# One wait per matmul: semaphore waits of TensorE dropped, moved to an earlier matmul, or moved to VectorE

## The reference: what is computed

```python
def _attn_ref(q, k, v):                       # q, k, v: 4 x 8 x 576 x 64
    scores = scale * np.matmul(q, k.transpose(0, 1, 3, 2))
    scores = np.where(mask, scores, -1000000000.0)   # block_i >= block_j, blocks of 64
    scores = scores - np.max(scores, axis=-1, keepdims=True)
    attn = np.exp(scores)
    attn = attn / (np.sum(attn, axis=-1, keepdims=True) + 1e-09)
    return np.matmul(attn, v)

def _moe_ref(x, w_in, w_out):                 # x: 2304 x 512, w_in: 512 x 2048
    h = x @ w_in
    g = np.where(h >= 1, h, np.where(h <= -1, 0.0, (h + 1) ** 2 / 4))
    return g @ w_out

def _moe2_ref(x, w_in, w_out):
    h = x @ w_in
    return (h * np.cos(h)) @ w_out
```

## Time and profile before

| | |
|---|---|
| median of 3 runs | 1044.91 us (1044.8 to 1045.8) |
| the profiled execution, its own time | 1051.79 us |
| its span, first to last instruction | 1049.6 us |
| PE busy | 1001.9 us, 95% of the span |
| DVE, ACT, POOL busy | 657.0, 590.8, 426.5 us (63%, 56%, 41%) |
| mean granted TensorE clock | 0.981 |

### The profile page before, as it was taken

How to read it: one execution, slowest core, us unless ns; L and a number is a source line. 1 busy time by engine, 2 the same in 40 slices (tenths; PEclk the granted TensorE clock), 3 DMA queues, 4 the chain that set the end, 5 groups by cost and what they waited for, 6 DMA issues and landing times.

```text
span 1049.6 us, 19879 instructions
## 1 busy us (share of the span) xinstructions
PE 1001.9 (95%) x7360; PEld 943.1 (90%) x7360; DVE 657.0 (63%) x1422; ACT 590.8 (56%) x1232; POOL 426.5 (41%) x446
## 2 busy tenths in 40 slices
PE   4688999999999999999999999999999999999997
PEld 3578999999999999999999998999999999999995
DVE  5567777766766767666732378656565555656553
ACT  5567776766666666666633356544444444445442
POOL 3559765555555554655522221222222222222211
PEclk9579999999999999999999999999999999999999
DMA  4335321221211212121200144010110101001000
GB/s 133 104 118 157 98 90 65 72 70 49 92 49 53 89 49 72 70 72 65 69 31 22 41 161 162 1 40 0 40 40 0 40 0 40 21 19 40 0 21 21
DMA packets 30886, 62.28 MB, mean 59 GB/s; under 512 B 3680, under 2 KB 11872, under 8 KB 30816
## 3 DMA queue, kind: packets, MB, share of 16 engines
q1 hardware_dynamic: 29664, 57.16, 17.1%
q10 hardware_dynamic: 1152, 4.19, 1.1%
HBM read 51.90 MB, written 9.44 MB: 58 GB/s over the span
## 4 chain that ended last, share of the span: by engine, by line
PE 79%; DVE 9%; ACT 5%; issue 3%; POOL 1%; DMA 1%; ACTq 0%; POOLq 0%; DVEq 0%
PE hidden L1090 33%; PE acc L1107 18%; PE acc L1115 12%; PE heads_out L1036 4%; PE scores L1001 4%; PE turned L1019 3%; PE scores L1002 3%; DVE neg_max L800 1%; PE heads_out L1019 1%; DVE x_lo L879 1%; PE hidden L1073 1%; DVE wout_lo L865 1%; DVE work L885 1%; ACT probs L616 1%; DVE pt_lo L817 1%
## 5 line engine op out<-in xcount | busy, mean ns | idle before, releaser
L543 POOL TENSOR_TENSOR g_lo<-work,g_hi 128x512 fp32r<-128x512 f32 x144 | 187.9, 1305 | 450.7 <-ACT g_hi L713 450.7
L1090 PE MATMUL hidden<-x_hi,win_hi 128*128 128x256 f32 x1136 | 323.5, 285 | 2.8 <-DVE work L912 1.2
L1090 PE MATMUL hidden<-x_hi,win_lo 128*128 128x256 f32 x1136 | 317.9, 280 | 0.0
L1090 PE MATMUL hidden<-x_lo,win_hi 128*128 128x256 f32 x1136 | 317.9, 280 | 0.0
L1090 PEld LDWEIGHTS hidden<-x_hi,win_hi 128*128 128x128 f32 x1136 | 214.3, 189 | 7.6 <-issue 2.0
L1090 PEld LDWEIGHTS hidden<-x_lo,win_hi 128*128 128x128 f32 x1136 | 214.2, 189 | 3.3
L1090 PEld LDWEIGHTS hidden<-x_hi,win_lo 128*128 128x128 f32 x1136 | 216.4, 190 | 0.0
L1115 PE MATMUL acc<-g_hi,wout_hi 128*128 128x256 f32 x576 | 167.4, 291 | 0.3 <-ACT y_stage L696 0.3
L1115 PE MATMUL acc<-g_lo,wout_hi 128*128 128x256 f32 x576 | 160.6, 279 | 0.0
L1115 PE MATMUL acc<-g_hi,wout_lo 128*128 128x256 f32 x576 | 160.5, 279 | 0.0
L513 POOL TENSOR_SCALAR probs<-probs,row_inv 64x576 f32<-64x576 f32 (+2 forms) x160 | 107.4, 675 | 121.6 <-DVE row_inv L812 120.8
(11 more groups left out here) (91 smaller groups left out, 1830.1 us busy)
## 6 DMA issues: line engine op xcount, KB each, us to landing
qk_raw<-qk_late SPq DMA_DIRECT2D x32, 448.0 KB, 3.2
qk_raw<-qk_early SPq DMA_DIRECT2D x32, 256.0 KB, 2.6
v_raw<-v_late SPq DMA_DIRECT2D x32, 160.0 KB, 3.3
x_raw<-x_scratch SPq DMA_DIRECT2D x9, 512.0 KB, 3.5
out<-y_stage SPq DMA_DIRECT2D x36, 128.0 KB, 2.4
x_raw<-w_in SPq DMA_DIRECT2D x8, 512.0 KB, 3.6
y_stage<-w_out SPq DMA_DIRECT2D x8, 512.0 KB, 3.5
x_scratch<-y_stage ACTq DMA_DIRECT2D x8, 512.0 KB, 2.7
```

Source lines behind the costliest of these rows:

```text
L543: nc.gpsimd.tensor_tensor(g_lo[:, m % G_RING, :], work[:, m % 2, :], g_hi[:, m % G_RING, :], ALU.subtract).then_inc(g_lo_made, 1)
L1090: last = nc.tensor.matmul(into, w[:, p, c, half * P:(half + 1) * P], x[:, c, :], start=(i == 0), stop=(i == len(products) - 1))
```

## The change

Three kinds of edits, all of them about which instruction waits for what. No computing instruction is added, removed or put elsewhere.

1. Waits that another one implies are left out on PE: `score` waits for `q_lo_made` at its first tile only, and no longer for `k_lo_made`; instead DVE waits for `k_lo_made` ahead of `split_q`, so that `q_lo_made` tells of both. The waits for the exponential remain at the third tile, and at the first where the order of the slots does not imply them (`banks_seen`).
2. Waits of `turn_b` and `turn_c`, of `make_hidden` (for `hidden_read`) and of `use_hidden` (for `g_lo_made`, `wout_lo_made`) move to one or two matmuls ahead of where they stood; `heads_read` and `v_lo_made` move from `weigh` to the transposes in part.
3. In the second layer the waits for each half of the weights (`half_lo_made`) are reduced to the last half that is made.

```diff
@@ split_q, DVE @@
             def split_q(n):
+
+                dve.wait_ge(k_lo_made, n + 1)
                 dve.wait_ge(q_hi_made, n + 1)
@@ score, PE @@
-                pe.wait_ge(q_lo_made, n + 1)
-                pe.wait_ge(k_lo_made, n + 1)
-
-                if late(n):
-                    pe.wait_ge(exp_made, first_tile(n) + (2 if i == 4 else 0))
-                elif n > ALONE:
-                    pe.wait_ge(exp_made, first_tile(n - 1) + e + 1)
-                elif n > 1:
-                    pe.wait_ge(exp_made, first_tile(n - 1 if n < ALONE else n))
+
+
+                if e == 0:
+                    pe.wait_ge(q_lo_made, n + 1)
+                    if not banks_seen(n):
+                        pe.wait_ge(exp_made, first_tile(n))
+                elif e == 2:
+                    pe.wait_ge(exp_made, first_tile(n) + 2)
@@ turn, PE @@
-                if e == 1:
-                    pe.wait_ge(heads_read, n)
-                elif e == 2:
-                    pe.wait_ge(pt_lo_made, first_turn(n) + 1)
-                elif user_before(n) >= 0:
-                    pe.wait_ge(pt_lo_made, first_turn(user_before(n) + 1))
...
+                    if not late(n) and c == 1 and user_before(n) >= 0:
+                        pe.wait_ge(heads_read, user_before(n) + 1)
+                    if kind(n) == 1 and c == 2:
+                        pe.wait_ge(v_lo_made, n + 1)
...
+            def turn_ahead(n, k):
+
+                for m, j in near(n, k):
+                    if late(m) and j == slot_of("turn_b", m):
+                        pe.wait_ge(heads_read, m)
+                    if late(m) and j == slot_of("turn_c", m):
+                        pe.wait_ge(pt_lo_made, first_turn(m) + 1)
+
             def weigh(n):
+
+
                 pe.wait_ge(pt_lo_made, first_turn(n) + (3 if late(n) else 1))
-                pe.wait_ge(v_lo_made, n + 1)
-                if user_before(n) >= 0:
-                    pe.wait_ge(heads_read, user_before(n) + 1)
+                if kind(n) == 0:
+                    pe.wait_ge(v_lo_made, n + 1)
@@ make_hidden, PE @@
-                if half == 0:
-                    pe.wait_ge(hidden_read, PAIRS * t + m + 1)
...
+                    if i == len(products) // 2 - 1:
+                        ahead_of_half(beside, 2 * u)
...
+                    if i == len(products) - 2 and ahead is not None:
+                        ahead()
+                    if i == len(products) - 1:
+                        ahead_of_half(beside, 2 * u + 1)
@@ tile, PE @@
-                    if second and (u % 4 == 0):
-                        for h in range(2):
-                            if s == 0:
-                                pe.wait_ge(half_lo_made[0][h], PAIRS - 1)
-                                pe.wait_ge(half_lo_made[1][h], PAIRS - 2)
-                            if s == PAIRS - LAG - 1:
-                                pe.wait_ge(half_lo_made[0][h], PAIRS)
-                            if s == PAIRS - 2:
-                                pe.wait_ge(half_lo_made[1][h], PAIRS)
+
+
+                    if second and u == 4 * (PAIRS - LAG - 1):
+                        pe.wait_ge(half_lo_made[1][1], PAIRS - 1)
+                    if second and u == 4 * (PAIRS - LAG) + 1:
+                        pe.wait_ge(half_lo_made[1][1], PAIRS)
```

More of the change, by code:

```diff
@@ L113, in user_before, with banks_seen @@
     return n - 2 if n < ALONE else n - 1
+def banks_seen(n):
+    before = n - 2 if n < ALONE else n - 1
+    last = "inv_c" if late(before) else "inv_b"
+    return n < 2 or slot_of(last, before) - sum(slots_of(m) for m in range(before, n)) <= slot_of("q_lo", n)
 def near(n, k):
@@ L1008, in turn @@
                 pe.wait_ge(probs_made, first_tile(n) + e + len(tiles))
-                if e == 1:
-                    pe.wait_ge(heads_read, n)
-                elif e == 2:
-                    pe.wait_ge(pt_lo_made, first_turn(n) + 1)
-                elif user_before(n) >= 0:
-                    pe.wait_ge(pt_lo_made, first_turn(user_before(n) + 1))
                 at = 0
-                for i, j in ([(0, 0), (1, 0), (1, 1)] if not late(n) else [(tiles[0], j) for j in range(tiles[0] + 1)]):
+                chunks = [(0, 0), (1, 0), (1, 1)] if not late(n) else [(tiles[0], j) for j in range(tiles[0] + 1)]
+                for c, (i, j) in enumerate(chunks):
                     q = rows_of(i)
+                    if not late(n) and c == 1 and user_before(n) >= 0:
+                        pe.wait_ge(heads_read, user_before(n) + 1)
+                    if kind(n) == 1 and c == 2:
+                        pe.wait_ge(v_lo_made, n + 1)
                     last = nc.tensor.transpose(turned_of(n, e)[:, at:at + q], probs_chunk(n, i, j), ident[0:q, 0:q])
@@ L1063, in beside_half, with ahead_of_half @@
                         attention(n, k)
+            def ahead_of_half(beside, half):
+                if beside:
+                    for n, k in beside[half]:
+                        turn_ahead(n, k)
             def begin_hidden(c):
@@ L1077, in begin_hidden, with hidden_ahead, use_ahead, make_hidden @@
                         last.then_inc(hidden_made, 1)
-            def make_hidden(t, m, half, beside=None, u=0):
+            def hidden_ahead(t, m):
+                pe.wait_ge(hidden_read, PAIRS * t + m + 1)
+            def use_ahead(t, p, first):
+                if p == 0:
+                    pe.wait_ge(g_lo_made, PAIRS * t + p + 1 + 2)
+                elif first:
+                    pe.wait_ge(wout_lo_made, p + 1)
+            def make_hidden(t, m, half, beside=None, u=0, ahead=None):
                 p = m % PAIRS
-                if half == 0:
-                    pe.wait_ge(hidden_read, PAIRS * t + m + 1)
                 into = hidden[:, m % H_BANKS, half * TOK:(half + 1) * TOK]
@@ L1093, in make_hidden, with use_hidden @@
                     last.then_inc(hidden_made, 1)
-            def use_hidden(t, p, half, second, beside=None, u=0):
-                if half == 0:
+            def use_hidden(t, p, half, second, beside=None, u=0, ahead=None):
+                if half == 0 and p == 0:
+                    pe.wait_ge(acc_read, t + 1)
+                elif half == 0:
                     pe.wait_ge(g_lo_made, PAIRS * t + p + 1 + 2)
-                    if p == 0:
-                        pe.wait_ge(acc_read, t + 1)
                 slot = p % G_RING
@@ L1105, in use_hidden @@
                         for i, (w, g) in enumerate(parts):
+                            if a == 1 and i == 1 and ahead is not None:
+                                ahead()
                             at = half * TOK + a * P
@@ L1113, in use_hidden @@
                         for i, (w, g) in enumerate(parts):
+                            if d == KC // 2 - 1 and i == 2:
+                                ahead_of_half(beside, 2 * u)
+                            if d == KC - 1 and i == 1 and ahead is not None:
+                                ahead()
+                            if d == KC - 1 and i == 2:
+                                ahead_of_half(beside, 2 * u + 1)
                             into = acc[:, d // 2, (d % 2) * TOK:(d % 2 + 1) * TOK]
@@ L1123, in tile, with ahead_of @@
                 heads = beside is not None
+                first = heads and t == 0
+                def ahead_of(u):
+                    s = u // 4
+                    if u == UNITS:
+                        return (lambda: hidden_ahead(t + 1, LAG)) if next_tile else None
+                    if u == made_at(s, heads) - 1 and (s + LAG < PAIRS or next_tile):
+                        return lambda: hidden_ahead(t, s + LAG)
+                    if u == (made_at(s, heads) + 1 if made_at(s, heads) == 4 * s + 1 else 4 * s) and (first or s == 0):
+                        return lambda: use_ahead(t, s, first)
+                    return None
                 for u in range(UNITS):
@@ L1138, in tile @@
                             if to_second and m >= PAIRS and half == 0:
-                                for h in range(2):
-                                    pe.wait_ge(half_lo_made[0][h], m - PAIRS + 1)
-                            if heads and t == 0 and m < PAIRS and half == 0:
+                                pe.wait_ge(half_lo_made[0][1], m - PAIRS + 1)
+                            if first and m < PAIRS and half == 0:
                                 pe.wait_ge(win_lo_made, m + 1)
-                            make_hidden(t, m, half, beside, u)
+                            make_hidden(t, m, half, beside, u, ahead_of(u + 1))
                     else:
-                        if heads and t == 0 and half == 0:
-                            pe.wait_ge(wout_lo_made, s + 1)
-                        use_hidden(t, s, half, second, beside, u)
+                        if first and s == 0 and half == 0:
+                            pe.wait_ge(wout_lo_made, 1)
+                        use_hidden(t, s, half, second, beside, u, ahead_of(u + 1))
```

(2 more changed lines are left out.)

## The result

The changed kernel takes 1146.06 us in the median of 4 runs (1144.07 to 1151.93), the kernel before 1044.86 us. The ratio is 1.0975, with a 95% interval of 1.0949 to 1.1001: 101 us slower, where 60 were forecast and 1130 us was the upper end of the range. The direction, the place and the size of the stall were right; the number of the clock's falls and the cost of a wait moved in the early items were not.

A forecast was written before the change was run, and what follows sets the result against it. PE was taken to bound the kernel, busy 1001.9 of 1049.6 us. Stalls 54.7 + early items 2 + clock 8 - saved waits 4 = 60.7 us, on the median 1044.9, gave 1105.6, said as 1105; range 1070 to 1130.

The forecast's parts named there:

- Part 1, "DVE stands still for 2.5 us": In each late item DVE stands still 2.5 us ahead of `split_q`, waiting for `k_lo`; near 75 us in the sum.
- a fixed price: DVE's 2.5 us stop, two POOL instructions of 1.04 + 1.41 us, is paid 32 times, once in every late item.
- Part 1, "18 x 2.1 + 13 x 1.3 = 54.7 us": PE's stalls at 31 pairs of late items: 18 lose 2.1 us in the mean, 13 lose 1.3.
- Part 1, the early items, 2 us for `k_lo`: In items 0, 15, 21 and 32 the score starts about 0.5 us later each: 2 us.
- Part 2, "I take 5, 8 us": PE's clock falls behind 5 of the stalls in late items, 1.6 us each: 8 us added.
- rival A: Same stalls in late items, but the clock falls at all 31, 50 us in place of 8: 1147 us, chance 8%.
- Part 3, moved waits at 0: PE's waits moved by one or two matmuls, and `heads_read` moved from `weigh` to the transposes, cost 0.
- Part 3, 4 us saved: In late items seven separate PE waits of 51 ns go or join weight loads: 4 us saved, at most 11.4.
- The sum's own base: The profiled execution, 1051.8 us, would become 1112.5; the median of the runs stands 6.9 us lower, at 1044.9.

The follow-up runs named there:

- only_k: The kernel before with one edit: DVE's `split_q` waits for `k_lo_made` and PE's `score` no longer does; 1126.80 us, ratio 1.0783.
- q_late: The changed kernel with `split_q` of late items put behind `pt_lo` in DVE's order, the wait for `k_lo_made` staying on DVE; 1071.57 us.
- the undoing runs: The changed kernel with the `k_lo_made` wait back on PE, 1055.67 us; also early `v_lo_made` back at `weigh`, 1047.35; also `heads_read`, 1045.72.
- the two fill runs: The changed kernel with ten or five added matmuls ahead of each `turn_c`'s wait for `pt_lo`; 1123.64 us with ten, 1130.05 us with five.
- before_again: The kernel before, unchanged, profiled a second time; an execution of 1045.34 us.

## Why the prediction was right in kind and wrong in size

- **Part 1, "DVE stands still for 2.5 us"**: right. 32 times, 76.2 us in the sum (near 75 forecast), 2.4 us in the mean, released by `k_lo`. That it is "a fixed price" was wrong: `normalise` got 0.28 us shorter (last section).
- **Part 1, "18 x 2.1 + 13 x 1.3 = 54.7 us"**: right. PE's wait for `pt_lo` grew from 2.0 to 55.9 us, its time not busy by 51.7; in `only_k` it waits 54.8 us, 31 times. `q_late` shows that the path is the one named, through `pt_lo`. That the sum comes out so close is partly luck, since the shorter `normalise` and the later start of the score behind `pt_lo` cancel (0.3 us each in item 53).
- **Part 1, the early items, 2 us for `k_lo`**: small, as said. `only_k` has 126 us there against 125.
- **Part 2, "I take 5, 8 us"**: this step failed, the term of the sum for the clock. It took 43 us: 21 falls in the late items, four of them of double length, so 25 times the 1.7 us that a fall costs. The price was about right (1.6 forecast, though its own working, 14 x 3.41 / 32, gives 1.5). The number was wrong: it was reached by counting only stalls of 2.0 us and more and then taking a third of them. Once the items no longer run alone the trace of before has one fall, and from one fall no shortest length can be read. In the changed kernel all eight stops of PE of 2.0 us and more bring a fall, and so do 14 of the 19 from 1.3 to 2.0 us. The match of 1146 with rival A's 1147 is partly chance: A had 50 us of clock and none of the 10 us of the next point.
- **Part 3, moved waits at 0**: the wait for `v_lo_made`, which moves from `weigh` to the transposes beside the one for `heads_read`, was not costed; it takes 8.3 us. The 0 for `heads_read` itself can't be told from the 1.6 us measured.
- **Part 3, 4 us saved**: nothing can be measured.
- **The sum's own base**: the profile of before was of the slower kind of execution. The forecast was a difference put on the median, so it did no harm there; it would have, had the second layer's spacing been read as the cost of its waits.

Put together for the profiled executions: 51.7 (idle time) + 43 (clock) + 11 (early items) = 106, of the 107 us between 1151.93 and 1045.34. Between the medians it is 101 in the place of 60.7, of which the undoing runs give 90.4 (`k_lo`), 9.9 (`v_lo`, `heads_read`) and 1.5 (the rest, 1045.72 against 1044.25, which its interval does not tell from zero).

Open: why the clock falls behind one stop and not behind a longer one, the 7 us in each of the two fill runs, and where the 6 us lie by which the profiled execution of the changed kernel is above its median (not in the loop: its tiles take 43.95 us).

## What to carry to other kernels

A wait that is moved to another engine "because it is implied" must be costed by what that engine has queued behind it: here 0.5 us of work had to wait for 2.4 us in the mean, and PE needed what stood one or two places further on. Moving one instruction in that engine's order took back four fifths of the loss. A wait that is already fulfilled cost PE nothing that could be measured here, so there was little to win from the start; and stops of PE that come again and again have to be priced with the clock: here 43 us came on top of 52.

## What the hardware showed that was not expected

**Short stops bring the clock down.** At the row that ends a stop of 1.31 us, and in the stretches behind it, the changed kernel shows 18 matmuls in 3.40 us at 0.51:

```profile
627.59 0.39 PE L1129 MATMUL hidden<-x_hi,win_lo 128*128 128x256 f32 x1 [1.31 <-DVE pt_lo L826]
```

```profile
629.40:632.80 3.40, 3.40 (x18) 3.40 (x16) 1.73 (x7) 0.69 (x3) 1.86 (x2) 0.51 0.26 89
```

A longer stop, 1.97 us, brought no fall:

```profile
323.17 0.39 PE L1162 MATMUL acc<-g_hi,wout_lo 128*128 128x256 f32 x1 [1.97 <-DVE pt_lo L826]
```

```profile
323.00:327.00 4.00, 3.83 (x28) 3.55 (x29) 3.50 (x10) 1.41 (x5) 0.00 (x0) 1.00 0.38 142
```

Of the 27 stops of 1.3 us and more in the late items, 22 have a fall while they last or within 2 us of their end (the last of these falls lies behind the stretch whose 21 were counted above); the other five, 1.34 to 1.97 us long, have none. The Trainium skill ("TensorE: Matmul & The Clock Gate", HAM oscillation) warns of idle gaps longer than the two shown here. The trace does not agree: the shortest stop with a fall behind it is the one of 1.31 us, and the measurement decides.

**POOL's `normalise` is slower beside `split_q`, and not beside DVE's other work.** `normalise` of a third tile, in the late items of `before_again`, of the changed kernel and of `q_late`:

```profile
L513 POOL TENSOR_SCALAR probs<-probs,row_inv 64x576 f32<-64x576 f32 x31 | 31.7, 1024 | 25.0 <-DVE row_inv L812 24.6
```

```profile
L520 POOL TENSOR_SCALAR probs<-probs,row_inv 64x576 f32<-64x576 f32 x31 | 22.9, 740 | 25.6 <-DVE row_inv L821 25.1
```

```profile
L520 POOL TENSOR_SCALAR probs<-probs,row_inv 64x576 f32<-64x576 f32 x31 | 23.0, 743 | 25.2 <-DVE row_inv L821 24.9
```

1024 ns with DVE's `split_q` beside it, 740 ns with DVE waiting: in the changed kernel DVE's stop is 0.28 us shorter than the trace of before would have it. In `q_late` DVE is not idle there in a third of the items, but works on a clamp, an activation or `pt_lo`, and `normalise` keeps its 0.74 us:

```profile
434.74 0.74 POOL L520 TENSOR_SCALAR probs<-probs,row_inv 64x576 f32<-64x576 f32 x1 [2.19 <-DVE row_inv L821]
434.57 0.66 DVE L899 TENSOR_TENSOR work<-hidden,work 128x512 f32<-128x512 f32 x1
```

So it is `split_q` that makes the difference. It alone of these reads both its inputs from SBUF, the others read at least one from PSUM; whether that is the reason was not tried.
